# k's transposes one step ahead in the recurrence, and no products with the zero state in the first chunk

## The reference

```python
cur = einsum(u * k[t], v[t])            # outer product, 48 x 48
y[t] = r[t] @ (state + cur)
state = w[:, None] * state + outer(k[t], v[t])
```

## Time and profile before

| what | value |
|---|---|
| median of 3 runs | 698.47 us |
| the profiled execution, its own time | 699.52 us |
| its span, first to last instruction | 697.7 us |
| TensorE matmul (PE), busy | 686.7 us, 98% of the span |
| TensorE weight load (PEld) | 623.7 us, 89% |
| VectorE (DVE) | 381.7 us, 55% |
| ScalarE (ACT) | 323.8 us, 46% |
| GpSimd (POOL) | 141.2 us, 20% |

### The profile page before, as it was taken

How to read it: one execution, slowest core, us unless ns; L and a number is a source line. 1 busy time by engine, 2 the same in 40 slices (tenths; PEclk the granted TensorE clock), 3 DMA queues, 4 the chain that set the end, 5 groups by cost and what they waited for, 6 DMA issues and landing times.

```text
span 697.7 us, 13712 instructions
## 1 busy us (share of the span) xinstructions
PE 686.7 (98%) x5072; PEld 623.7 (89%) x5072; DVE 381.7 (55%) x788; ACT 323.8 (46%) x704; POOL 141.2 (20%) x190
## 2 busy tenths in 40 slices
PE   7999999999999999999999999999999999999998
PEld 5888888879999999899999999999999989998997
DVE  5677667678777777666543443343434333434333
ACT  5777777735555555554433333233333333324222
POOL 8757966543232321100000000000000000000000
PEclk9999999999999999999999999999999999999999
DMA  7888876718666668320023004000500050001001
GB/s 137 186 201 198 186 170 153 238 39 294 232 216 211 223 208 279 104 25 1 1 60 32 1 1 84 7 1 0 92 1 0 1 91 1 0 1 47 0 1 45
DMA packets 135161, 65.70 MB, mean 94 GB/s; under 512 B 110724, under 2 KB 130696, under 8 KB 135104
## 3 DMA queue, kind: packets, MB, share of 16 engines
q1 hardware_dynamic: 131088, 60.13, 33.6%
q0 software_dynamic: 2560, 4.60, 2.1%
q10 hardware_dynamic: 1456, 0.20, 0.2%
HBM read 53.37 MB, written 12.48 MB: 94 GB/s over the span
## 4 chain that ended last, share of the span: by engine, by line
PE 94%; DVE 2%; POOL 1%; issue 1%; DMA 1%; ACT 0%; another core or an unknown queue 0%; DVEq 0%; ACTq 0%; POOLq 0%
PE bank_A L1038 8%; PE bank_A L1039 8%; PE bank_A L1037 8%; PE bank_L L1037 4%; PE bank_L L1039 4%; PE bank_L L1038 4%; PE bank_P L1039 4%; PE bank_P L1038 4%; PE bank_P L1037 4%; PE bank_kT L1038 4%; PE bank_kT L1039 4%; PE bank_kT L1037 4%; PE bank_A L954 4%; PE bank_YT L1039 3%; PE bank_YT L1038 3%; PE bank_YT L979 3%
## 5 line engine op out<-in xcount | busy, mean ns | idle before, releaser
L1595 DVE TENSOR_TENSOR g_lo<-g,g_hi 128x512 fp32r<-128x512 f32 x96 | 66.5, 692 | 67.1 <-ACT g_hi L824 67.1
L824 ACT ACTIVATE g_hi<-g 128x512 fp32r<-128x512 f32 x96 | 60.7, 632 | 73.1 <-DVE g L1593 73.1
L1593 DVE SCALAR_TENSOR_TENSOR g<-cut,bank_A 128x512 f32<-128x512 f32 x60 | 41.2, 687 | 76.4 <-ACT cut L821 76.4
L821 ACT ACTIVATE cut<-bank_A 128x512 f32<-128x512 f32 x60 | 35.8, 597 | 94.2 <-PE bank_A L1039 93.7
L1039 PE MATMUL bank_A<-mT_hi,wi_lo 128*128 128x512 f32 x180 | 71.0, 394 | 0.0
L1038 PE MATMUL bank_A<-mT_lo,wi_hi 128*128 128x512 f32 x180 | 70.9, 394 | 0.0
L1037 PE MATMUL bank_A<-mT_hi,wi_hi 128*128 128x512 f32 x180 | 70.0, 389 | 0.0
L658 ACT ACTIVATE bank_A<-ident,own 128x128 f32<-128x128 f32 x188 | 58.1, 355 | 23.7 <-DVE A_sb L1293 18.7
L1593 DVE SCALAR_TENSOR_TENSOR g<-cut,bank_kT 128x512 f32<-128x512 f32 x36 | 24.7, 687 | 67.5 <-ACT cut L821 67.5
L821 ACT ACTIVATE cut<-bank_kT 128x512 f32<-128x512 f32 x36 | 21.5, 597 | 70.5 <-PE bank_kT L1039 70.5
L1037 PE MATMUL bank_kT<-mT_hi,wi_hi 128*128 128x512 f32 x108 | 42.1, 389 | 0.9 <-DVE mT_lo L1586 0.9
(11 more groups left out here) (333 smaller groups left out, 1807.1 us busy)
## 6 DMA issues: line engine op xcount, KB each, us to landing
raw<-in_moe_w_dram SPq DMA_DIRECT2D x24, 512.0 KB
raw<-in_moe_w_dram SPq DMA_DIRECT2D x7, 1536.0 KB
r_in<-in_r_dram SPq DMA_DIRECT2D x24, 192.0 KB, 3.6
v_in<-in_v_dram SPq DMA_DIRECT2D x24, 192.0 KB, 4.2
x_scratch<-y_sb SPq DMA_DIRECT2D x24, 192.0 KB, 2.3
k_in<-in_k_dram SPq DMA_DIRECT2D x23, 192.0 KB, 3.8
m_in<-x_scratch SPq DMA_DIRECT2D x20, 192.0 KB, 5.5
out_dram<-o_sb SPq DMA_DIRECT2D x10, 384.0 KB, 2.8
```

The costliest lines, as they stand in the source:

```text
L821: eng.activation(cut[f % 2][:, :], p_H[f % 3][:, :], ACT.Relu, bias=0.5, scale=1.0 / 6.0).then_inc(s_cut, 1)
L824: eng.activation(g_hi[f % 4][:, :], g[f % 2][:, :], ACT.Copy).then_inc(s_ghi, 1)
L1593: eng.scalar_tensor_tensor(g[f % 2][:, :], cut[f % 2][:, :], 1.0, p_H[f % 3][:, :], ALU.min, ALU.mult).then_inc(s_g, 1)
L1595: eng.tensor_tensor(g_lo[f % 4][:, :], g[f % 2][:, :], g_hi[f % 4][:, :].bitcast(F32), ALU.subtract).then_inc(s_glo, 1)
```

## The change

TensorE transposes r of step n + 1 where it did, but k of step n + 2, in a function of its own, behind the products for the state and ahead of A times v (step 0 does k of steps 1 and 2). ScalarE copies kT of step n + 1 ahead of both halves of the seeds. In the first chunk, where the state is zero, the product with the state is left out; A times v then starts the accumulation, `s_Yst` counts from the second chunk on, and VectorE waits for the zeroed state where TensorE did.

```diff
@@ ScalarE, step
                 if n < NT - 1:
+                    k_transposed(*after)
                     diagonal(n + 1, 0)
-                    k_transposed(*after)
                     diagonal(n + 1, 1)
@@ TensorE, transposes
                 m.then_inc(s_rtr, 1)
+                if n < 2:
+                    k_transposes(b, c)
+
+            def k_transposes(b, c):
+                n = c * B + b
                 if n == 0:
                     busy(2)
                     eng.wait_ge(s_wk, 2)
...
@@ TensorE, step
-                if c == 0:
-                    eng.wait_ge(s_nought, b + 1)
                 wait(eng, s_state, n - B + 1)
                 wait(eng, s_xT, n)
-                for q in range(NPAIR):
+                for q in range(NPAIR if c else 0):
                     for o in range(2):
...
-                m.then_inc(s_Yst, 1)
+                if c:
+                    m.then_inc(s_Yst, 1)
                 if c < NC - 1:
                     products(b, n)
+                if n < NT - 2:
+                    k_transposes((b + 2) % B, c + (b + 2) // B)
                 eng.wait_ge(s_vin[b], 16 * (c + 1))
...
-                                       start=False, stop=h == H - 1, skip_group_check=True)
+                                       start=c == 0 and q == 0, stop=h == H - 1, skip_group_check=True)
@@ VectorE, r_transposed
-                wait(eng, s_Yst, n - 1)
+                wait(eng, s_Yst, n - 1 - B)
@@ VectorE, update
-                eng.wait_ge(s_Yst, n + 1)
+                if n < B:
+                    eng.wait_ge(s_nought, b + 1)
+                wait(eng, s_Yst, n + 1 - B)
```

## The result

| | before | after |
|---|---|---|
| median of 5 runs, us | 698.47 (697.96 to 700.05) | 702.30 (702.00 to 703.87) |
| ratio to before | | 1.0052, 95% interval 1.0040 to 1.0063 |
| profiled execution / its span, us | 699.52 / 697.7 | 702.00 / 700.2 |

The change costs 3.8 us. The forecast was 5.1 more than before, 703.6 us; 702.3 lies in its range, on the side it named.

The account below looks back on a forecast made before the run. The prediction took the spacing of PE's instructions, with no waits, to bound steps 4 to 22. It summed -0.1 us for the first chunk and +5.2 for steps 4 to 21 to +5.1: 703.6 us, range 701.0 to 705.6.

Parts of the forecast that it names:

- P to K, over P to V: From next-state products to the moved k transposes: next start after 0.20 instead of 0.05 us, +0.15 per step.
- inside K and K to V: Within the moved k transposes +0.05 us; from them to the A-times-v products +0.09 us.
- inside V: Within the A-times-v products, now behind a change of shape: 1.01 instead of 0.98 us, +0.03.
- The rival with one gap: Change behind the short next-state products costs less: 0.12 to 0.20 us per step, +2.5, 701.0 us; chance 0.14.
- between the full array and a shape split by columns: Such changes between PE groups delay the next start to about 0.2 us after the last, in both directions.
- Steps 4 to 21: Twelve steps at 0.32, four chunk ends at 0.28, steps 20 and 21 at 0.14 each: together +5.2 us.
- The first chunk: Steps 0 to 3 lose the state products, 4.1 us of PE work, but give only 0.1 us.
- The loop of 4.55 through ScalarE: First chunk: with kT's copy ahead of the seeds, the seeds' loop falls from 5.02 to 4.55 us.
- wait for k_dec in step 2: PE waits for GpSimd's k_dec of step 4; k transposes start about 25.0, step 4 at 31.1 instead of 31.25.
- Other edits: VectorE's looser waits, zeroed states, step 22 without k transposes, DMA and GpSimd's k_dec timing: each costed at nothing.
- GpSimd was not late: k_dec at chunk ends holds by 0.4 us, cost nothing; rival of lateness: 705.6 us at 0.5 late, chance 0.05.
- I carry the shift through unchanged: Behind step 22 everything follows by data, so the +5.1 us reaches the end of the kernel.

Follow-up runs that it names:

- e4: Kernel before plus one full-width identity transpose between next-state products and A-times-v products in steps 4 to 19: 703.31 us, ratio 1.0090.
- e1: Kernel after with k's transposes and ScalarE's order put back, only the zero-state products left out: 697.73 us, ratio 1.0019.
- e6: Kernel after with the 3 MB load of w_out moved behind m_first's load: 702.44 us, ratio 1.0057.
- v4: Kernel after with only GpSimd's scatters moved behind the next step's k_dec: 703.71 us, one execution.
- e3: Kernel before plus one full-width identity transpose between the r and k transposes in steps 4 to 19: 699.07 us, ratio 1.0027.
- e5: Kernel before with the 3 MB load of w_out moved behind m_first's load: 699.08 us, ratio 1.0003.
- v1: Kernel after with k's transposes moved between the gate's products and the products with the state: 704.63 us, ratio 1.0078.
- v2: v1 with GpSimd's scatters behind the next step's k_dec and step 4's k transposes behind step 2's A-times-v products: 700.10 us, ratio 1.0024.
- e2: Kernel before with k's transposes moved and kT's copy ahead of the seeds, zero-state products kept: 702.86 us, ratio 1.0087.
- v6: v5 with the load of w_out moved behind m_first's load as well: 699.34 us, ratio 1.0002.
- v3: Kernel after with only step 4's k transposes moved behind step 2's A-times-v products: 708.06 us, one execution.
- v5: v2 with k's transposes directly behind x's transposes, ahead of the gate's products: 699.31 us, ratio 1.0019.

## Why the prediction was right

**The changes of shape: right in kind, one term too large.** The sum named four terms for a step with S and P. Step 5 has for them:

| term | predicted | measured |
|---|---|---|
| P to K, over P to V | +0.15 | 0.60 - 0.50 = +0.10 |
| inside K and K to V | +0.05 + 0.09 | 0.58 - 0.44 = +0.14 |
| inside V | +0.03 | 1.02 - 0.98 = +0.04 |
| step | +0.32 | +0.28 to 0.29 |

The term that was mis-sized is "P to K: 0.20 instead of the 0.05". The 0.20 was read behind V, and it contains V's own distance from one pair of matmuls to the next, about 0.10 with 128 columns. Behind P, with 48 columns, that distance is 0.05, and the next start comes after 0.15, in the kernel after as in e4. What the change adds is 0.10 behind either. The prediction says so itself ("about 0.1 us over the matmul's own spacing") but does not use it in its sum. The rival with one gap was wrong: the change adds as much behind short matmuls as behind long ones. The term makes 16 x 0.05 = 0.8 us too much; the others give 0.2 of it back, so steps 4 to 21 make 0.6 of the 1.3 us by which the forecast was too high.

The prediction speaks of a change "between the full array and a shape split by columns". That is too narrow: S to P keeps its 64 columns and changes the rows alone, 64 to 128, and costs the same 0.20.

**Steps 4 to 21.** Twelve full and four reduced steps, as told: 12 x 0.285 + 4 x 0.23 + 2 x 0.15 = 4.64 against 5.2. From the A of step 4 to that of step 22 the two profiles differ by 4.04 + 0.54 = 4.58, which the 5.19 of step 13 before makes 0.08 too small. The last steps of a chunk lose 0.05 less than the others; the forecast had 0.04.

**The first chunk.** The loop of 4.55 through ScalarE came out (4.54, 4.55), e1 shows that without the copy ahead S is worth nothing, and PE did wait for k_dec in step 2. Step 0, which transposes k of two steps, is 0.10 us longer; the sum had no term for it, and the wait in step 2 swallows it. The price of that wait was over-estimated: k_dec was written from 23.50 and not from 23.89, since k's load ended 0.39 earlier in this execution, and K began 0.06 behind it, where 25.0 had been put. So A of step 4 was at 30.71 instead of 31.1. In e6 and v4, which do the same in this chunk, k_dec begins at 23.21 and 23.33 and that A is at 30.42 and 30.52: a time set by a load moves by some tenths from one execution to another (23.11 to 23.89 in the 14 profiles, 23.45 to 23.89 in those of before, e3, e4 and e5), and it should have been given a range. This is 0.4 us more of the 1.3.

**Other edits.** Of those costed at nothing no row shows a cost. Step 22 is 0.43 us shorter without a K (5.35 for 5.78), and PE waits 1.10 us for y_sb in place of 0.67, so X of step 23 is late by 4.03, as step 22's A was by 4.04. GpSimd was not late (v4).

**Behind step 22.** "I carry the shift through unchanged" held for the medians, 3.8 us of 4.04 (the last 0.2 of the 1.3), and not for the two profiles, which end 2.5 apart. The timeline before, end of step 23, has a stall that the profile after lacks:

```profile
140.45 0.63 PE L990 MATMUL bank_YT<-A_sb,v_in 128*48 128x128 f32 x6 [0.44 <-issue]
140.54 0.18 DVE L1375 TENSOR_TENSOR pick<-bank_P,choice 128x16 f32<-128x16 f32 x1 [2.40 <-remote]
...
141.12 0.38 ACT L723 ACTIVATE xT<-bank_YT 128x256 f32<-128x256 f32 x1 [1.91 <-PE bank_YT L990]
```

VectorE's row there is this one after:

```profile
143.05 0.18 DVE L1383 TENSOR_TENSOR pick<-bank_P,choice 128x16 f32<-128x16 f32 x1 [0.86 <-PE bank_P L948]
```

And the windows of before, then of after, behind it:

```profile
146.00:150.00 4.00, 4.00 (x25) 4.00 (x25) 2.38 (x20) 1.71 (x5) 1.42 (x3) 0.57 0.11 37
```

```profile
146.00:150.00 4.00, 3.81 (x35) 3.33 (x34) 3.55 (x21) 3.07 (x8) 2.25 (x3) 1.00 0.33 102
```

Before, three engines stand still and the granted clock then falls to 0.57 of full; after, it stays full. By the transposes of L1045 (166.41 before; L1051, 168.40 after) the 4.04 us between the two profiles have become 1.99, so stall and clock together were worth 2.0 us there. A wait of 0.25 us for xg in the kernel after then brings the distance back to some 2.4.

This is no property of the change. The wait of VectorE at that row, 2.3 to 2.4 us, stands in the profiles of before, v1, v2, v4 and e5, and not in those of e1, e3 and e4, which have the kernel before's order of K. The clock falls behind step 23 in e2 and e3 too, without that wait (0.50 from 144 to 146 and from 140 to 142 us). Of the five executions of the kernel after, the profiled one has the highest mean clock, 0.999 against 0.995 to 0.998. In e5 stall and clock (0.61 in the same window, 1.00 in e6) come without the load of w_out, so that load is not their cause. What stops the engines is open.

## What to carry to other kernels

Before a group of matmuls is moved, look at the tile shapes of its old and its new neighbours: on a TensorE with no idle time, a full-width group put between two column-split ones pays at both sides, in every step, and the busy times don't show it. Put it among its likes. When you take the price of such a gap from a row elsewhere, take off the matmul's own distance first: here 0.10 us is added, behind 48 columns as behind 128. Work taken from the engine with the longest busy time is worth only what the loop through the other engines leaves (1.02 us cut, nothing gained), so find that loop first. Asking for an operand earlier is a new deadline for the engine that makes it, and where a wait grows to a microsecond or two, the fallen clock behind it can cost as much again.

## What was unexpected of the hardware

- A change of shape adds 0.10 us to the distance between starts, behind either length measured: 0.15 for 0.05 behind 48 columns, 0.20 for 0.10 behind 128. It also makes the group behind it longer by 0.04 to 0.05. The weight loads of the new shape are not seen to begin before its first matmul. A single transpose put between P and V cost 0.40 us, of which 0.11 was the transpose.
- After waits of 1 to 2 us in otherwise full stretches the granted clock was 0.50 (1.2 GHz) for some 3 us (v1, behind 1.84 us; v6, behind 1.08), but in v3 for 17 us; after the waits of 1.18 and 1.10 us in the kernel after it stayed at 1.00. The length of the wait alone does not tell.
- Engines can stand still although the groups they wait for have ended: in v6's step 21 ScalarE for 1.1 us and VectorE for 0.5 longer than before, with DMAs nearly idle (share 0.02); in v5 such a stall came with DMAs full (1.05 from 122 to 124 us). In step 21 it came in each of the four profiles with GpSimd's scatters moved and in none of the ten others. At the end of step 23 VectorE stood for 2.3 to 2.4 us in five profiles of fourteen.
